# First MLP block: its normalisation, transposes and first weight split moved into attention's last rounds

## What is computed

```python
scores = q_rot @ k_rot.T / 8;  attn = softmax(scores);  o = attn @ v
x = o.transpose(0, 2, 1, 3).reshape(4, 576, 512)
xn = (x - mean(x)) / sqrt(var(x) + 1e-6) * g_ln              # first MLP
x = x + relu(xn @ w_ch1) @ w_ch2                             # 512 -> 2048 -> 512
h = gelu(x @ w_in);  u, v = halves of h                      # second MLP
v = normalised v;  v = w_sg @ v + b_sg                       # over positions
out = x + (u * v) @ w_out
```

## Time and profile before

| | us |
|---|---|
| median of 3 runs | 949.27 |
| lowest and highest | 947.62, 951.3 |
| the profiled execution | 949.65 |
| its span, first to last instruction | 947.8 |
| PE busy, share of the span | 920.0, 97% |
| DVE busy | 512.4, 54% |
| ACT busy | 401.6, 42% |
| POOL busy | 261.2, 28% |

### The profile page before, as it was taken

One profiled execution on the slowest core, in us unless ns is written; L12 is line 12 of the kernel. 1 busy time (PEld: TensorE's weight loads), 2 busy tenths in 40 slices (PEclk: granted clock), 3 DMA queues, 4 the chain that ended last, 5 costly groups with the idle time before them and its releaser, 6 DMA issues.

```text
span 947.8 us, 15722 instructions
## 1 busy us (share of the span) xinstructions
PE 920.0 (97%) x5577; PEld 825.6 (87%) x5577; DVE 512.4 (54%) x907; ACT 401.6 (42%) x861; POOL 261.2 (28%) x241
## 2 busy tenths in 40 slices
PE   4999999999998799999999999999999999999998
PEld 3999999999997688889888888888888999989897
DVE  4899999999998544242221223132224663663623
ACT  3899999999996332211211211122123221312111
POOL 4989989989941000000000000000000100010100
PEclk9999999999999999999999999999999999999999
DMA  6243243243320332200000000003100001010011
GB/s 175 64 103 91 68 104 84 72 105 79 79 66 3 121 104 89 89 1 1 1 0 1 1 0 0 0 0 113 45 1 1 1 1 45 2 44 13 1 45 56
DMA packets 44966, 44.24 MB, mean 47 GB/s; under 512 B 14128, under 2 KB 34864, under 8 KB 44784
## 3 DMA queue, kind: packets, MB, share of 16 engines
q1 hardware_dynamic: 44480, 43.21, 16.3%
q10 hardware_dynamic: 432, 0.30, 0.1%
HBM read 28.81 MB, written 4.72 MB: 35 GB/s over the span
## 4 chain that ended last, share of the span: by engine, by line
PE 94%; DVE 3%; ACT 1%; DMA 1%; issue 1%; SPq 0%; ACTq 0%; DVEq 0%
PE hid_ps L1595 21%; PE acc_ps L1609 21%; PE ring_ps L1505 9%; PE scores_ps L1441 7%; PE wide_ps L1719 6%; PE ring_ps L1452 6%; PE wide_ps L1701 5%; PE bank_ps L1733 5%; PE bank_ps L1681 5%; PE scores_ps L1434 2%; PE ring_ps L1388 2%; PE ring_ps L1463 1%; PE ring_ps L1518 1%; PE ring_ps L1473 1%; PE xT_ps L1532 1%; PE bank_ps L1654 1%
## 5 line engine op out<-in xcount | busy, mean ns | idle before, releaser
L1595 PE MATMUL hid_ps<-xT,W1s 128*128 128x512 f32 (+1 forms) x960 | 211.8, 371 | 3.2 <-DVE xT L1148 3.2
L1609 PE MATMUL acc_ps<-W2s,hid 128*128 128x512 f32 x864 | 210.5, 391 | 0.0
L1595 PEld LDWEIGHTS hid_ps<-xT,W1s 128*128 128x128 f32 x960 | 169.8, 190 | 35.6 <-DVE xT L1148 3.2
L1609 PEld LDWEIGHTS acc_ps<-W2s,hid 128*128 128x128 f32 x864 | 160.5, 188 | 32.6 <-DVE hid L1228 0.2
L1228 DVE SCALAR_TENSOR_TENSOR hid<-hid_ps,hid 128x512 fp32r<-128x512 f32 (+1 forms) x80 | 51.0, 638 | 254.0 <-ACT hid L914 254.0
L914 ACT ACTIVATE hid<-hid_ps 128x512 fp32r<-128x512 f32 (+1 forms) x80 | 44.4, 555 | 305.4 <-PE hid_ps L1595 305.4
L1071 DVE TENSOR_REDUCE nmax<-scores_ps 128x1 f32<-128x576 f32 x144 | 107.2, 754 | 16.0 <-PE scores_ps L1441 10.7
L824 ACT ACTIVATE E<-scores_ps,nmax 128x576 f32<-128x576 f32 x128 | 95.9, 750 | 9.3 <-DVE nmax L1071 8.5
L781 POOL TENSOR_TENSOR rstd<-ve,power 128x1 f32<-128x1 f32 x18 | 14.6, 814 | 306.1 <-DVE ve L1299 306.1
L1080 DVE TENSOR_TENSOR prob_lo<-ring_ps,prob_hi 128x512 fp32r<-128x512 f32 x144 | 95.5, 682 | 2.6 <-ACT prob_hi L838 2.6
L838 ACT ACTIVATE prob_hi<-ring_ps 128x512 fp32r<-128x512 f32 x144 | 85.9, 615 | 6.0 <-PE ring_ps L1452 4.3
(11 more groups left out here) (138 smaller groups left out, 1442.2 us busy)
## 6 DMA issues: line engine op xcount, KB each, us to landing
swapped_k<-stack SPq DMA_DIRECT2D x64, 144.0 KB, 2.5
w_raw<-in_w SPq DMA_DIRECT2D x32, 256.0 KB, 3.0
qk_raw<-in_k SPq DMA_DIRECT2D x16, 256.0 KB, 2.7
v_raw<-in_v SPq DMA_DIRECT2D x16, 256.0 KB, 2.7
qk_raw<-in_q SPq DMA_DIRECT2D x15, 256.0 KB, 2.8
out<-out_sb SPq DMA_DIRECT2D x14, 256.0 KB, 2.2
w_raw<-in_win SPq DMA_DIRECT2D x4, 512.0 KB, 4.6
rotary<-rotary_table SPq DMA_DIRECT2D x2, 576.0 KB, 5.0
```

The source lines that it names most:

```text
L1595: mm = nc.tensor.matmul(hid_ps[:, f % 2, 0:cols], W1s[:, slot1(f), w, c, :], xT[:, x, c, 0:cols], start=first, stop=(c == DC - 1 and x == 1))
L1609: mm = nc.tensor.matmul(acc_ps[:, t, :], hid[:, f % 2, x, P * t:P * t + P], W2s[:, slot2(f), w, :], start=(f == 0 and x == 0 and w == 0), ...
```

## The change

- SP: the DMAs of the weights' first two chunks are issued in round 14, behind that round's key swaps, instead of behind all rounds.
- POOL: `inverse_std(0)` in round 13 (with pair 12) instead of 15. New `first_weights`: in round 15 it splits W1 of chunks 0 and 1 and W2 of chunk 1, once the last pair's Q and K are transposed; in round 16, once all scores are made, W2 of chunk 0. ACT and DVE no longer split these.
- DVE: statistics, mean and variance of block 0 in round 12 instead of 15; the four `normalise` instructions one by one in round 14, at the four places of round 14 at which the statistics stood in round 15; `xT_low(0, c)` between the subtractions of round 16.
- ACT: `xT_high(0, c)` between the copies of round 16.
- PE: x of block 0 is transposed in round 16, chunks 0 and 1 ahead of the key tails, 2 and 3 behind them, into the banks of the score buffers (`acc_ps`). `hidden(0, 0)` runs in round 17, right behind the last product with V and ahead of `transpose_o`. The tails of the output are transposed behind it, then `hidden(0, 1)`.
- The ring's banks are allocated in the order 3, 0, 1, 2, so that `hid_ps` lies over banks 3 and 0. `project(0, 0)` also waits for four low splits of weights, `hidden(0, f)` for the ring's last reads (`wait_bank_done`).

The diff, cut:

```diff
-        ring_ps = [psum(att_ps, f"ring_ps{n}", [P, 512]) for n in range(4)]
+        ring_ps = {n: psum(att_ps, f"ring_ps{n}", [P, 512]) for n in (3, 0, 1, 2)}
...
             if isinstance(n, int) and n == 0:
-                return (hid_ps[:, 1], xT_ps[:, 0], xT_ps[:, 1], hid_ps[:, 0])[c]
+                return acc_ps[:, c]
...
# SP, end of body(r)
+                if is_round(r, PAIRS - 2):
+                    for f in range(2):
+                        load_weights(f)
...
-            for f in range(NF):
-                if f >= 2:
-                    sp.wait_ge(w_lo, 2 * (f - 1))
+            for f in range(2, NF):
+                sp.wait_ge(w_lo, max(2 * (f - 1), 4))
+                load_weights(f)
...
# POOL
-                if is_round(p, PAIRS - 2):
+                if is_round(p, PAIRS - 4):
                     inverse_std(0)
...
+            def first_w1(f):
+                pool.wait_ge(w_in[f], 32)
+                nc.gpsimd.tensor_copy(W1s[:, slot1(f), 0, :, :], w1_raw[:, f, :, :]).then_inc(w_hi, 1)
+                pool.wait_ge(w_hi, (1, 2)[f])
+                nc.gpsimd.tensor_tensor(W1s[:, slot1(f), 1, :, :], w1_raw[:, f, :, :], W1s[:, slot1(f), 0, :, :].bitcast(f32),
+                                        ALU.subtract).then_inc(w_lo, 1)
...
+            def first_weights(p):
+                if is_round(p, PAIRS - 1):
+                    wait_filled(pool, p, ("Q", 0), ("Q", 1), ("K", 0), ("K", 1), ("TL", 0))
+                    first_w1(0)
+                    first_w1(1)
+                    first_w2(1)
+                if is_round(p, PAIRS):
+                    pool.wait_ge(scores, PAIRS * NQK)
+                    first_w2(0)
...
                 v_low(r - 1)
+                first_weights(r)
...
# ACT, body(r)
                 copy_stack(r, 1, 1)
+                first_block_high(r, 0)
                 prob_high(r - 1, "KT", 0)
...
                 prob_high(r - 1, "G1", 1)
+                first_block_high(r, 1)
...
                 prob_high(r - 1, "G2", 1)
+                first_block_high(r, 2)
                 copy_o(r - 1, 0, 1)
+                first_block_high(r, 3)
...
+                if isinstance(n, int) and n == 0:
+                    act.wait_ge(v_lo, PAIRS)
                 act.wait_ge(xT_done, n * DC + c + 1)
...
# DVE
-                if is_round(r, PAIRS - 1):
-                    tile_statistics(0, 0)
+                first_block(r, 0)
                 maximum(r, 0)
                 prob_low(r - 1, "G1", 0)
+                first_block_low(r, 0)
...
-                if is_round(r, PAIRS - 1):
+                if is_round(r, PAIRS - 4):
                     mean_variance(0)
                 prob_low(r, "G3", 0)
                 sum_o(r - 1, 1, 0)
                 maximum(r, 8)
-                if is_round(r, PAIRS - 1):
-                    normalise(0)
...
+            def first_block(r, t):
+                if is_round(r, PAIRS - 4):
+                    tile_statistics(0, t)
+                if is_round(r, PAIRS - 2):
+                    normalise(0, (t,))
+            def first_block_low(r, c):
+                if is_round(r, PAIRS):
+                    xT_low(0, c)
...
# PE
+            def wait_bank_done(b):
+                pe.wait_ge(freed[b], PAIRS * len(bank_order[b]))
...
                     if isinstance(n, int) and n == 0:
-                        b = (1, 2, 3, 0)[c]
-                        pe.wait_ge(freed[b], PAIRS * len(bank_order[b]))
+                        pe.wait_ge(expd, count(exp_order, pair(PAIRS - 1), 7 + c // 2))
                     else:
+                        if isinstance(n, int) and n == 1 and c < 2:
+                            wait_bank_done((1, 2)[c])
                         head_wait(pe, xT_lo, n, DC, c - 1)
...
                 times_v(r - 2, 1, 0, range(2, NTT))
+                if is_round(r, PAIRS + 1):
+                    hidden(0, 0)
...
                 make_stack(r, 1, 1)
+                if is_round(r, PAIRS):
+                    transpose_x(0, range(0, 2))
                 transpose_key_tails(r - 1)
+                if is_round(r, PAIRS):
+                    transpose_x(0, range(2, DC))
...
                 if isinstance(n, int) and n == 0:
-                    pe.wait_ge(w_lo, 2 * f + 2)
+                    pe.wait_ge(w_lo, 2 * f + 2 if f >= 2 else f + 1)
+                    if f < 2:
+                        wait_bank_done((3, 0)[f])
...
                         pe.wait_ge(tails_merged, B)
+                        pe.wait_ge(w_lo, 4)
...
+            rounds(pe, body, (-2, 1))
+            transpose_o_tails()
             def mlp1_block(n):
-                hidden(n, 0)
+                if not (isinstance(n, int) and n == 0):
+                    hidden(n, 0)
```

More of the change, by code:

```diff
@@ L638, in body, with load_weights @@
                 swap_keys(r + 1, 0)
-            rounds(sp, body, (-2, 2))
-            for f in range(NF):
-                if f >= 2:
-                    sp.wait_ge(w_lo, 2 * (f - 1))
+                if is_round(r, PAIRS - 2):
+                    for f in range(2):
+                        load_weights(f)
+            def load_weights(f):
                 sp.dma_start(w1_raw[:, f % 2, :, :], w1_v[:, :, f * P:(f + 1) * P]).then_inc(w_in[f % 2], 16)
                 sp.dma_start(w2_raw[:, f % 2, :], w2_v[f]).then_inc(w_in[f % 2], 16)
+            rounds(sp, body, (-2, 2))
+            for f in range(2, NF):
+                sp.wait_ge(w_lo, max(2 * (f - 1), 4))
+                load_weights(f)
             sp.wait_ge(w_lo, 2 * NF)
@@ L756, in _, with first_w2 @@
             pool.wait_ge(zeroed, 2)
+            def first_w1(f):
[4 more added lines that the diff above has]
+                                        ALU.subtract).then_inc(w_lo, 1)
+            def first_w2(f):
+                nc.gpsimd.tensor_copy(W2s[:, slot2(f), 0, :], w2_raw[:, f, :]).then_inc(w_hi, 1)
+                pool.wait_ge(w_hi, (4, 3)[f])
+                nc.gpsimd.tensor_tensor(W2s[:, slot2(f), 1, :], w2_raw[:, f, :], W2s[:, slot2(f), 0, :].bitcast(f32),
+                                        ALU.subtract).then_inc(w_lo, 1)
+            def first_weights(p):
[7 more added lines that the diff above has]
+                    first_w2(0)
             def body(r):
@@ L946, in mlp2_weights_high, with first_block_high @@
                     nc.scalar.activation(wsT[TAIL:P, 0, NT, :], wsT[0:TAIL, 0, NT, :].bitcast(f32), ACT.Copy).then_inc(wsT_hi, 1)
[L948 to L951, removed]
+            def first_block_high(r, c):
+                if is_round(r, PAIRS):
+                    xT_high(0, c)
+            rounds(act, body, (-2, 0))
             blocks(act, mlp1_block)
@@ L1134, in mean_variance, with normalise @@
                 nc.vector.tensor_tensor(ve1[:, 0:nt], mv1[:, 0:nt, 1], ve1[:, 0:nt], ALU.add).then_inc(mean_var, 1)
-            def normalise(n):
+            def normalise(n, tiles=None):
                 nt = block_tiles(n)
@@ L1139, in normalise @@
                 head_wait(dve, xT_done, n, DC, 0)
-                for t in range(nt):
+                for t in tiles or range(nt):
                     last = nc.vector.tensor_scalar(xhat[:, t, :].rearrange("p (h c) -> p h c", h=HP), block_tile(n, t),
                                                    mv1[:, t, 0:1], rstd1[:, t:t + 1], ALU.subtract, ALU.mult)
-                last.then_inc(xhat_s, 1)
+                if t == nt - 1:
+                    last.then_inc(xhat_s, 1)
             def xT_low(n, c):
@@ L1170, in body @@
                 prob_low(r - 1, "G2", 1)
+                first_block_low(r, 2)
                 sum_o(r - 1, 0, 1)
-                if is_round(r, PAIRS - 1):
-                    tile_statistics(0, 2)
+                first_block_low(r, 3)
+                first_block(r, 2)
                 maximum(r, 4)
@@ L1178, in body @@
                 sum_o(r - 1, 0, 0)
[L1179 to L1180 removed]
+                first_block(r, 3)
                 prob_low(r, "G0", 0)
@@ L1202, in weights_low @@
                                         ALU.subtract).then_inc(w_lo, 1)
[L1204 to L1207, removed]
+            rounds(dve, body, (-2, 0))
             dve.wait_ge(rinv_kept_s, PAIRS)
@@ L1571, in body @@
                 make_stack(r + 1, 0, 1)
[L1573 to L1581, removed]
             def hidden(n, f):
@@ L1611, in project, with transpose_o_tails @@
                 mm.then_inc(fc2, 1)
+            def transpose_o_tails():
+                for h in range(2):
+                    pe.wait_ge(o_tail_kept[h], 16 * PAIRS)
+                for b in range(B):
+                    for hp in range(HP):
+                        mm = nc.tensor.transpose(scores_flat[b // 2][0:TAIL, 512 * (b % 2) + P * hp:512 * (b % 2) + P * hp + P],
+                                                 o_tail[:, HP * b + hp, :], ident[:, :])
+                    mm.then_inc(tails_ps, 1)
+            rounds(pe, body, (-2, 1))
+            transpose_o_tails()
```

(3 more changed lines are left out.)

9 lines of the change are left out of this document (3 added, 6 removed).

## The result

| | before | after |
|---|---|---|
| median of the runs, us | 949.52 (4 runs) | 941.44 (4 runs) |
| lowest to highest | 947.62 to 951.3 | 940.78 to 943.21 |
| the profiled execution | 949.65 | 940.78 |
| its span | 947.8 | 939.0 |

The ratio of after to before is 0.9918, with a 95% interval from 0.9894 to 0.9942: 8 us, or 0.8%, faster. A second series gave 0.9917 (0.9902 to 0.9932).

What follows compares the result with a forecast made beforehand. PE was taken as the bound, with DVE only 1.35 us to spare. Gains of 2.9 (attention's end) and 8.4 (seam) less 2.9 net cost gave 8.4: 941.2 profiled, 940.8 median; range 937.0 to 946.5.

Steps and rivals of the forecast that it cites:

- Attention's end: With normalisation moved earlier, the last attention product ends at 307.5 instead of 310.41, before the net cost: gain 2.9 us.
- net cost: Rounds 12 to 15: 1.7 lost in round 12, 2.2 in round 14, 1.0 given back in 15: 2.9 us.
- The seam: Last attention product to first product into acc_ps: 7.9 us of PE work plus 0.2 wait instead of 16.5, gain 8.4.
- tails merge and low part: At the seam, DVE's merge and first hid_lo end near 315.4, as the second hidden product does; 0.2 us wait charged.
- The chunk 2 weights: Loads start at about 308 and land by 312; their split on ACT and DVE is hidden beside the second product.
- The clock: Seam: no clock fall, 1.8 of the 8.4 gained; the rival that it falls anyway gave 943.8, chance 0.10.
- Rounds 12 to 15: PE loses 1.7 in round 12, nothing in 13, 2.2 in 14; round 15 gives its 1.04 back.
- a wait of 0.4: Round 12: one lock wait on POOL between 0 and 1.44 us, taken as 0.4.
- no relief: Round 12: the 128x9 tensor_scalar gets no cheaper, unlike in round 15, where 0.76 us was saved.
- the lock waits: Round 14: normalise instructions wait for POOL between 0 and 5.8 us, taken as three medians of 0.76: 2.3.
- The slack of 1.4 per round: Loaded rounds: 1.4 us of added DVE work vanishes in slack, as taken from round 15 of the kernel before.
- The weights' part: Round 15: POOL, without an instruction there, splits weights in at most 8.6 us, hidden inside the round.

Runs made afterwards that it cites:

- the accumulating form: Changed kernel with each of block 0's four normalise instructions also writing the accumulator (a dummy; output off by a relative 0.47): median 941.23 us.
- The spread version: Changed kernel with statistics of two tiles each in rounds 12 and 13, mean and variance in 13, power one round later, normalise in round 15: 940.47 us.
- e8_eps_pool: Changed kernel with normalise in round 15 and block 0's 1e-6 added by POOL instead of DVE: 939.70 us, ratio 0.9896.
- r_after: The changed kernel run once more, unaltered, as the measure for follow-up runs: 941.58 us (940.98 to 943.82).
- e1_norm_round15: Changed kernel with block 0's four normalise instructions at the same places of round 15 instead of 14: 940.46 us, ratio 0.9906.
- e7_only_weights: Kernel before with only the weights moved (four transfers in round 14, POOL splits chunks 0 and 1): 947.8 us, ratio 0.9992.
- e11_second_half: Changed kernel with normalise in round 15, 1e-6 on POOL, accumulating 128x9 addition, statistics only at the later places of rounds 12 and 13: 939.64 us.
- e2_norm_end: Changed kernel with all four normalise instructions at the end of round 15, ahead of the write of Y, as before the change: ratio 0.9919.

## Why the prediction was right, point by point

The forecast was 940.8 for a median of 941.44, and 941.2 for a profiled execution of 940.78.

- **Attention's end.** The key tails' transposes were to start at 299.3 plus the 2.9 of net cost: 302.2; they start at 301.72. From there to the end of the last product 8.2 was forecast: 309.93 - 301.72 = 8.21. PE stayed last, as argued; x transposes filled the hole.
- **The seam.** 8.1 forecast from the last attention product to the first into acc_ps, 7.82 measured. That DVE's tails merge and low part end with the second hidden product held to 0.1. The chunk 2 weights came later than said (ACT waits 0.8 for them until 314.1, I had 312), behind cover all the same.
- **The clock.** At 1.00 throughout. The two profiles with a hole left ahead of 303 (1.46 us with all four at the end, 3.95 with the weights alone) show a lower one behind it (0.84, 0.71), as the earlier trace rows did. The price that I took from the earlier trace rows, 1.8 at the hidden product and some 1.2 ahead of it, is that of the profiled execution, and 34 of the 41 executions of before are about 2.4 slower than the seven whose clock did not fall. So this part of the gain comes in most executions and not in all.
- **Rounds 12 to 15.** Net 3.4 forecast at mark 15 (1.7 + 2.2 - 0.5), 3.2 measured in the first profile and 3.9 in the second. The terms were less good than the sum, and that the sum came so close in the first is in part luck. Rounds 12 and 13 cost 1.3 in the first profile and 2.1 in the second, by whether the variance's step waits for the end of one POOL instruction or of the next; I had 1.7, with a wait of 0.4 that was 0.6 or 1.4, and "no relief" where the 128x9 addition in fact fell from 0.91 to 0.15. Round 14 cost 2.4 (0.77 + 1.61) against 2.2; the lock waits were 1.9 (4.02 less 4 x 0.54), I had 2.3. What I hadn't priced is the other direction: POOL's six instructions on Q and K take 9.0 us instead of 8.4 there, and 8.5 with the accumulating form, so POOL waits for DVE too.
- **The slack of 1.4 per round.** This step was wrong in kind. The spread version shows that it isn't a sum per round; it gave the right size here since round 15 of before, from which it came, had the same instructions at the same places.
- **The weights' part.** "POOL has not one instruction in round 15, so it is hidden" was right for this change only because normalise had left the end of round 15. The run with the weights alone shows what the cover is worth: without it, the split costs 1.2 us of DVE and, in that profile, the clock. In size the term was too large: POOL's six instructions in round 15 took 5.8 us, where I had at most 8.6.

Shown by an experiment: the port's lock (the form and the place of the instructions changed alone), the hole's cause, the price of a microsecond of DVE, the variance step. Argued only: what the lower clock costs apart from the hole, since it comes in some executions and not in others; that the late keys are what PE waited for in round 15; and how the 4.9 us that neither part gives divide between the hole, x in round 16 and the order of the tails.

A version of the change that may be faster still is e8_eps_pool: normalise one round later, 1e-6 added by POOL. All its five runs (up to 940.55) lie under all six of r_after (from 940.98), though in another series; by the ratios to before, 0.9896 against 0.9917, the intervals overlap.

## What to carry to other kernels

When work is moved under another stage, ask per instruction whether it shares a port with what runs there: a small SBUF-to-SBUF instruction on DVE can cost a whole POOL instruction (the variance's step and tensor_scalar did, the reciprocal and the accumulating form did not), and the cure may be another form, another engine or a round in which POOL pauses, not less work. Measure the price of added work at its place: slack in one half of a loop body isn't to be had in the other. And a part whose cover is another part of the same change must not be judged, nor shipped, alone: here each of two parts was worth nothing clear of the spread, and the whole gave 8 us. And see which execution a profile is of: two of the profiles here are of the fastest and of the slowest of their kernel, and read alone they would have shown differences that the other executions don't bear out.

## What the runs showed of the hardware

- DVE's tensor_scalar (128x512, SBUF to SBUF) takes 0.53 to 0.54 us where it meets no POOL instruction and up to 1.79 beside one; in the accumulating form it took 0.79 to 0.80 in all four places. bn_stats took 0.67 to 0.68 in every place with POOL busy.
- Such waits come in steps of POOL's instruction: the variance step took 0.76 to 0.78 or 1.53 to 1.55 in otherwise equal executions, and PE's loss moved with it by 0.8 us. It may be a part of the spread between runs; only profiled executions show it.
- POOL casts 128x512 from f32 to fp32r in 0.61 to 0.62 us in the changed kernel, and subtracts two such tiles in 1.28 to 1.30. Beside a normalise instruction of DVE the same cast took 0.81 (e1_norm_round15, e7_only_weights) and the same subtraction 1.59 (e11_second_half).
- PE's waits of 1.46, 2.71 and 3.95 us in a dense stretch were each followed by a lower granted clock in the profiled executions (0.84, 0.82 and 0.71 over the next 9 to 11 us); a wait of 1.12 us in round 12 of r_after was not (1.00). The clock does not fall in every execution of the same kernel: over the whole span its mean was under 1.000 in one of four of e2_norm_end and in 34 of 41 of the kernel before.
